# Sixteen token sums of a two-layer MLP kernel move from VectorE's queue to GpSimd's

## The reference

```python
# attention, per chunk of 32 queries: 8 memory keys + 16 before + 32 + 8 after
scores = scale * np.matmul(q_c, k_full.transpose(0, 1, 3, 2))
a = np.exp(scores - np.max(scores, axis=-1, keepdims=True))
a = a / (np.sum(a, axis=-1, keepdims=True) + 1e-09)
out[:, :, c_start:c_end] = np.matmul(a, v_full)
...
x = attn_out.transpose(0, 2, 1, 3).reshape(3072, 512)
h = x @ w_in                                  # layer 1: 512 -> 2048
x = np.where(h > 0, h, np.exp(np.minimum(h, 0)) - 1) @ w_out   # -> 512
h = x @ w_in2                                 # layer 2
out = (s * np.maximum(h, 0) ** 2 + b) @ w_out2
```

## Time and profile before

| | us |
|---|---|
| median of three runs | 1129.36 |
| lowest, highest | 1125.82, 1129.99 |
| profiled execution, whole | 1129.36 |
| its span, first to last instruction | 1127.6 |
| TensorE busy | 1092.7 |
| VectorE busy | 816.1 |
| ScalarE busy | 782.0 |
| GpSimd busy | 364.6 |

### The profile page before, as it was taken

How to read it: one execution, slowest core, us unless ns; L and a number is a source line. 1 busy time by engine, 2 the same in 40 slices (tenths; PEclk the granted TensorE clock), 3 DMA queues, 4 the chain that set the end, 5 groups by cost and what they waited for, 6 DMA issues and landing times.

```text
span 1127.6 us, 18143 instructions
## 1 busy us (share of the span) xinstructions
PE 1092.7 (97%) x5787; PEld 873.3 (77%) x5787; DVE 816.1 (72%) x1226; ACT 782.0 (69%) x1842; POOL 364.6 (32%) x411
## 2 busy tenths in 40 slices
PE   8999898989999999999999999999999999999998
PEld 4677666767777777788787888888888888888886
DVE  5796686468867856887868968868747578566475
ACT  5897786677677657768758677677676476774574
POOL 7587889760012423105465023761000000000000
PEclk9899999999999999999999999999999999999999
DMA  9997999999798898979899689997696666776664
GB/s 192 240 280 223 360 340 354 346 326 330 223 284 268 235 262 260 311 221 385 290 351 350 204 307 338 338 338 255 193 302 209 195 195 190 217 220 194 191 196 155
DMA packets 203479, 300.71 MB, mean 267 GB/s; under 512 B 112760, under 2 KB 120952, under 8 KB 203384
## 3 DMA queue, kind: packets, MB, share of 16 engines
q1 hardware_dynamic: 203384, 299.55, 86.7%
HBM read 224.00 MB, written 75.50 MB: 266 GB/s over the span
## 4 chain that ended last, share of the span: by engine, by line
PE 74%; ACT 5%; DMA 5%; SPq 5%; POOL 4%; issue 3%; DVE 3%; ACTq 0%; POOLq 0%; DVEq 0%
PE ps L1032 37%; PE ps L1017 31%; DMA w_scratch<-w_new 3%; DMA w_ring<-w_scratch 2%; POOL w_new L829 2%; PE ps L926 2%; ACT ps L1117 1%; SPq L624 1%; ACT elu L1210 1%; PE ps L978 1%; PE ps L951 1%; ACT elu L1215 1%; PE ps L920 1%; SPq L623 1%; SPq L634 1%
## 5 line engine op out<-in xcount | busy, mean ns | idle before, releaser
L1017 PE MATMUL ps<-xc_hi,w_ring 128*128 128x512 f32 x1344 | 433.1, 395 | 8.8 <-ACT s L1183 6.0
L1032 PE MATMUL ps<-g_hi,w_ring 128*128 128x512 f32 x1344 | 420.4, 394 | 5.8 <-issue 3.0
L1017 PEld LDWEIGHTS ps<-xc_hi,w_ring 128*128 128x128 f32 x1344 | 252.3, 188 | 67.5 <-issue 6.7
L1032 PEld LDWEIGHTS ps<-g_hi,w_ring 128*128 128x128 f32 x1344 | 250.0, 189 | 62.2 <-issue 4.9
L1032 PE MATMUL ps<-g_lo,w_ring 128*128 128x512 f32 x672 | 263.1, 391 | 0.0
L1017 PE MATMUL ps<-xc_lo,w_ring 128*128 128x512 f32 x672 | 261.8, 390 | 0.0
L829 POOL TENSOR_TENSOR w_new<-w_raw,w_new 128x256 fp32r<-128x256 f32 x171 | 163.4, 963 | 256.6 <-ACT w_new L1264 254.5
L1529 DVE TENSOR_TENSOR g_lo<-X,g_hi 128x512 fp32r<-128x512 f32 x240 | 174.4, 731 | 30.0 <-ACT g_hi L1250 29.5
L1250 ACT ACTIVATE g_hi<-X 128x512 fp32r<-128x512 f32 x240 | 150.2, 630 | 56.6 <-PE ps L1032 53.7
L1032 PEld LDWEIGHTS ps<-g_lo,w_ring 128*128 128x128 f32 x672 | 126.8, 189 | 26.9
L1017 PEld LDWEIGHTS ps<-xc_lo,w_ring 128*128 128x128 f32 x672 | 126.3, 188 | 24.0
(11 more groups left out here) (125 smaller groups left out, 1307.9 us busy)
## 6 DMA issues: line engine op xcount, KB each, us to landing
w_ring<-w_scratch SPq DMA_DIRECT2D x332, 512.0 KB, 4.5
w_scratch<-w_new SPq DMA_DIRECT2D x171, 256.0 KB, 5.3
w_scratch<-att SPq DMA_DIRECT2D x45, 256.0 KB, 5.8
w_raw<-in_moe_w_in SPq DMA_DIRECT2D x16, 512.0 KB, 5.7
w_raw<-in_moe_w_out SPq DMA_DIRECT2D x16, 512.0 KB, 6.1
x_scratch<-y SPq DMA_DIRECT2D x12, 512.0 KB, 6.2
att<-x_scratch SPq DMA_DIRECT2D x12, 512.0 KB, 6.3
out<-elu SPq DMA_DIRECT2D x24, 256.0 KB, 4.3
```

The lines of the kernel that those rows point to most:

```text
L1017: last = nc.tensor.matmul(bank_of(st, st.i), w[:, a, cols], x[:, st.pi, kk, :], start=(st.pi in (P1, P5) and kk == 0 and n == 0), stop=(kk ...
L1032: last = nc.tensor.matmul(bank_of(st, d), w[:, a, cols], x[:, k % RING, :], start=(st.pi in (P1, P5) + (P4,) * (1 - st.gr) and st.i == 0 a ...
```

## The change

The eight sums of tile 1 and the eight of tile 2 leave VectorE's loop. GpSimd makes them in `sums_of_x`, called for tile 1 behind the preparation of weight sets 14 and 15, and for tile 2 behind set 19. Their order is half 0's P5, P6, P7, then half 1's, then P4 of both, where VectorE had made both halves of each kind in turn; `x_sum` is changed to that order. The operands, the buffers and the waits of each sum stay. The late sums, those of the second layer's tiles, stay on VectorE.

```diff
--- before.py
+++ after.py
@@ -241,8 +241,6 @@
 LOAD_AT = (88, 94)
 SPLIT_LATE = ((P1, 0, 99), (P1, 1, 100)) + tuple((pi, kk, 106 + 2 * i + kk) for i, pi in enumerate((P2, P5, P6, P7, P4, P3))
                                                  for kk in range(2))
-NEXT_SUMS = {106 + i: (pi, kk) for i, (pi, kk) in enumerate((pi, kk) for pi in (P5, P6, P7) for kk in range(2))}
-NEXT_SUMS.update({114: (P4, 0), 115: (P4, 1)})
 LATE_SUMS = 54
 LATE = [(pi, kk) for pi, kk, _ in SPLIT_LATE]
 OUT_BLOCKS = TOK // 128
@@ -564,7 +562,7 @@
 
         def x_sum(t, kk, pi):
             first = HEAD_SUMS + 8 * (t - 1)
-            return first + 2 * (P5, P6, P7, P4).index(pi) + kk + 1
+            return first + (7 + kk if pi == P4 else 3 * kk + {P5: 1, P6: 2, P7: 3}[pi])
 
         def sums_done(t, gr, pi, j):
             return 16 * (2 * t + gr) + SUMS.index((pi, j)) + 1
@@ -853,6 +851,23 @@
                 for m in ms:
                     split_w(m, P3)
 
+            def sums_of_x(t):
+                n = HEAD_SUMS + 8 * (t - 1)
+                for kk in range(2):
+                    pool.wait_ge(x_in[kk], 32 * t)
+                    x12, x22 = (x_from(t, kk, pi) for pi in (P7, P3))
+                    x11 = x_from(t, kk, P1)
+                    t2 = x_from(t, kk, P6)
+                    pool.wait_ge(x_lo_done, x_count(t) + x_index(t, kk, P1) + 1)
+                    nc.gpsimd.tensor_tensor(x11, x12, x11, ALU.subtract).then_inc(x_sums, 1)
+                    pool.wait_ge(x_sums, n + 3 * kk + 1)
+                    nc.gpsimd.tensor_tensor(t2, x22, x11, ALU.subtract).then_inc(x_sums, 1)
+                    nc.gpsimd.tensor_tensor(x12, x22, x12, ALU.subtract).then_inc(x_sums, 1)
+                for kk in range(2):
+                    x21, t2 = x_from(t, kk, P2), x_from(t, kk, P6)
+                    pool.wait_ge(x_lo_done, x_count(t) + x_index(t, kk, P6) + 1)
+                    nc.gpsimd.tensor_tensor(t2, x21, t2, ALU.subtract).then_inc(x_sums, 1)
+
             def sums_of_head(c):
                 lo, hi = HEAD_COLS[c]
                 b11, b12, b21, b22 = (xh[:, kt:kt + 2, h * HALF + lo:h * HALF + hi]
@@ -875,8 +890,10 @@
             for m in range(4, PAIR):
                 prepare((m,))
             prepare(sets_of(PAIR))
+            sums_of_x(1)
             for m in range(SETS, SETS + 4):
                 prepare((m,))
+            sums_of_x(2)
             for m in range(SETS + 4, 2 * SETS):
                 prepare((m,))
 
@@ -1413,24 +1430,6 @@
                     to, a, b = t4, x21, t2
                 nc.vector.tensor_tensor(to, a, b, ALU.subtract).then_inc(late_sums, 1)
 
-            def next_x_sum(t, kk, pi):
-                x11, x12, x21, x22 = (x_from(t, kk, b) for b in (P1, P7, P2, P3))
-                t2 = x_from(t, kk, P6)
-                if pi == P5:
-                    dve.wait_ge(x_in[kk], 32 * t)
-                    dve.wait_ge(x_lo_done, x_count(t) + x_index(t, kk, P1) + 1)
-                    to, a, b = x11, x12, x11
-                elif pi == P6:
-                    dve.wait_ge(x_sums, x_sum(t, kk, P5))
-                    to, a, b = t2, x22, x11
-                elif pi == P7:
-                    dve.wait_ge(x_sums, x_sum(t, kk, P5))
-                    to, a, b = x12, x22, x12
-                else:
-                    dve.wait_ge(x_lo_done, x_count(t) + x_index(t, kk, P6) + 1)
-                    to, a, b = t2, x21, t2
-                nc.vector.tensor_tensor(to, a, b, ALU.subtract).then_inc(x_sums, 1)
-
             def lo_x(t, kk, pi):
                 dve.wait_ge(x_hi_done, x_count(t) + x_index(t, kk, pi) + 1)
                 nc.vector.tensor_tensor(xc_lo[:, pi, kk, :], x_from(t, kk, pi), xc_hi[:, pi, kk, :].bitcast(F32),
@@ -1604,10 +1603,6 @@
                 for xt, kk, pi in x_split_at(g - 1):
                     lo_x(xt, kk, pi)
                 t, s = divmod(g, PER_TILE)
-                for xt in range(1, TPL):
-                    if g - PER_TILE * (xt - 1) in NEXT_SUMS:
-                        pi, kk = NEXT_SUMS[g - PER_TILE * (xt - 1)]
-                        next_x_sum(xt, kk, pi)
                 if TPL <= t + 1 < TILES and 0 <= s - LATE_SUMS < 8:
                     late_x_sum(t + 1, (s - LATE_SUMS) % 2, (P5, P7, P6, P4)[(s - LATE_SUMS) // 2])
                 for n, at in woven_at(g):
```

## The result

The changed kernel takes 1138.39 us (median of 5 runs) against 1129.99 us (median of 5): ratio 1.0067, 95% interval 1.0039 to 1.0097. The ratio is above the 0.5% bound (the interval reaches down to 0.4%); I had forecast no change, with a range up to 1133.5 us. The profiled execution is a short one, 1132.67 us with a span of 1130.3.

What follows compares the result with a forecast made beforehand. TensorE, busy 97% of the span, was taken to bound the kernel. From 1129.4 us, -0.3 at passage 0-1 and +0.7 at passage 1-2 gave 1129.8 us, range 1126.0 to 1133.5.

Steps and rivals of the forecast that it cites:

- What bounds the kernel: Whole kernel: TensorE, busy 97% of the span; less VectorE work is worth only TensorE's waits at the two passages.
- the worth of the relief: Both passages: VectorE's queue gets 4.8 us shorter at each, but TensorE gains 0.7 us at most.
- Added work: GpSimd at both passages: sixteen 128x512 subtractions, 1.27 to 1.69 us each, fitting its idle time; costed at nothing.
- weight preparation: GpSimd behind the sums: second-layer weight differences run later, a lo cut at most about 1 us later; costed at nothing.
- semaphores: Sums at both passages: 1.4 us each including the semaphore, and no new wait for SyncE.
- lateness of the sums: Both passages: sums come in time, 7.4 and 5.0 us early at passage 1-2; nothing on TensorE's path.
- The port as the unknown: SBUF port shared by VectorE and GpSimd: each moved sum can hold up VectorE's next cut for up to 1.27 us.
- rival 2: Both passages: the port lock falls wholly on VectorE, +3.7 us, 1133.1 us; chance 0.10.
- Bound of VectorE's delay: Up to step 111's g_lo cut: lock costs TensorE at most 0.5 us at passage 0-1, 3.2 at passage 1-2.
- the halving: Both passages: half of VectorE's standing time taken, leaving it 0.4 us late at passage 0-1, 0.7 at passage 1-2.
- Rival 3: Passage 1-2: GpSimd starves at the port, sums take 3.84 us and come late, +6.7 us, 1136.1 us; chance 0.03.
- Rival 1: Both passages: VectorE always goes first and the gaps close, -0.7 us, 1128.7 us; chance 0.10.

Runs made afterwards that it cites:

- paced halves: All sixteen sums on GpSimd as in the changed kernel, but spread over TensorE's steps and each cut into two 256-column instructions; 1129.59 us, 0.9996 against the kernel before.
- P4 only: Against the kernel before, only the four P4 sums move to GpSimd, the other twelve stay on VectorE; timed 1131.87 us, ratio 1.0025.
- paced kernel: The changed kernel with most GpSimd sums held back by waits on TensorE's step count; 1129.73 us, ratio 1.0010 against the kernel before.
- second comparison: The changed kernel, nothing further altered, timed again against the kernel before; 1136.84 us, ratio 1.0067.

## Why the prediction was wrong

**What bounds the kernel, and the worth of the relief: right as far as the runs tell.** I had at most 0.7 us to be had; of the 0.54 us at passage 0-1 the paced halves got 0.34 back, and no timed kernel is clear of no gain.

**Added work, weight preparation, semaphores, lateness of the sums: right.** The sums took 1.3 to 1.8 us (forecast 1.3 to 1.7) and were early: ScalarE never waited for one at either passage. The weight cut behind them came 1 us later, for which SyncE alone waited (0.3 us). "P4 only" has the same queue behind its sums and its phases are within 0.3 us of those before or shorter.

**The port as the unknown: right in kind, wrong in size.** It is rival 2, with 5.9 to 6.9 us in place of its 3.7. The step that failed is "Bound of VectorE's delay", at two points.

First, the place and the cover. I took the delay at the g_lo that step 111 reads, where the slack is 2.1 us (passage 0-1), and let the PSUM work (3.2 us in 298.3 to 308.1) and three removed sums (1.8 us) pay for it. But VectorE works in order, and four of the five PSUM instructions and all three sums stood behind the first five cuts. These met five holds of 0.9 to 1.1 us, so the fifth cut ended 4.9 us late. The slacks of the kernel before are read from these rows (line 1360 is the copy, 920 the attention piece; 491.76 is step 109's cut, 493.28 its first products):

```profile
303.94 0.69 DVE L1360 COPY att<-ps 128x512 f32<-128x512 f32 x1
...
491.76 0.69 DVE L1529 TENSOR_TENSOR g_lo<-X,g_hi 128x512 fp32r<-128x512 f32 x1
...
304.98 0.62 PE L1032 MATMUL ps<-g_hi,w_ring 128*128 128x512 f32 x2
...
306.45 0.63 PE L920 MATMUL ps<-may_see,chunk_of 3*96 3x512 bf16 x2
...
493.28 0.61 PE L1032 MATMUL ps<-g_hi,w_ring 128*128 128x512 f32 x2
```

The down phase of tile 0 begins at 263.18 us before and at 259.23 after, and the times are compared from there. The fifth cut had ended at 302.22 and step 108 began at 304.98, 2.8 us of slack: 4.9 - 2.8 = 2.1 us on TensorE, and step 108 began 2.2 us late. The copy for attention had ended at 304.63 and the piece began at 306.45, 1.8 us of slack; the copy ended 4.8 us late (one removed sum had paid 0.6, a sixth hold took 0.5), which makes 3.0 of the 3.1 us measured. My bound for this passage was 0.5. Nor did the bound hold at the cut for which I had worked it out: step 111's cut (307.79) ended 3.6 us late and not at most 2.6, since PSUM work ran beside a sum for about 0.9 us (the end of a copy at 294.32 and the add at 303.09) and not for 3.2.

At passage 1-2 the down phase lost 3.2 to 3.8 us against a bound of 3.2, but that the number is near is luck: I had it at step 111, and TensorE waited at steps 108 and 109 and no more behind them. Step 109's cut had 0.8 us of slack (it had ended at 492.45) and, counted from the phase's start (458.26 before, 457.36 after), ended 4.5 us late: 3.7 us on TensorE.

Second, the halving. I took half of the standing time, because VectorE's chains had kept GpSimd out for 3.84 us in the earlier trace rows. Every one of the six sums held up one cut, five of them for nearly their whole length: these cuts read 1.60 to 1.79 us where I had written 1.0 to 1.3, and VectorE was busy 5.7 us longer where I had written the same or less. The forecast (-0.3 for passage 0-1, +0.7 for passage 1-2) fell with it.

**The order of the two effects.** The first sum stood on VectorE at 303.34; on GpSimd the sums began at P1's lo cut, 4.9 us earlier against VectorE's own queue (298.4 in the clock of the kernel before), and ran back to back in its densest row of cuts. I had counted their being early (7.4 us at passage 1-2) as safety. The paced kernel begins its first sum just as early and spreads the others, and its loss is gone from the first down phase: so the cost is the row of holds.

**The rivals.** Rival 3 (starving sums) didn't come: no sum took over 1.8 us. Rival 1 (relief only) is what the paced halves come near to in their phases, but the timing can't part that from no change. The chance of 0.04 for slower was too small: rival 2's price was called a bound, and was worked out for one cut of each passage, with a cover that wasn't there.

**Still open.** The phases explain 5.9 to 6.9 us, the timing says 7.6 (5.1 to 9.9 in the second comparison); whether the rest is scatter of the first 260 us or something else the profiles don't settle.

## What to carry to other kernels

Before instructions go to GpSimd, list VectorE's instructions with two SBUF inputs in the stretch where they will run: each may wait for nearly one whole GpSimd instruction that reads SBUF, and later PSUM work or removed instructions don't pay for it, because the queue is in order. Check the slack after every one of them and not at the end of the stretch. If the work must go there, spread it so that undisturbed cuts come between, or cut it in pieces: here a piece of 512 columns (1.27 us alone) cost a cut 1.1 us, one of 256 columns (0.74 us alone) 0.54 us.

## What the runs showed that I had not expected

Two engines that both read SBUF alternated, one GpSimd sum, one cut, for the whole row, 1.7 us a pair; in the earlier trace rows the same kind of pair let VectorE run five instructions before GpSimd got its turn. What decides which of the two happens I don't know, and no run here tells.

GpSimd's plain writes to SBUF didn't touch VectorE at all: eighteen memsets of 0.58 us each over cuts of 0.68 us.
